# Starting the work area of SBUF 32 bytes later

## The reference

```python
for t in range(S):
    state = gamma * state + einsum('bhd,bhe->bhde', k[:, :, t], v[:, :, t])
    y[:, :, t] = scale * einsum('bhd,bhde->bhe', q[:, :, t], state)
x = y.transpose(0, 2, 1, 3).reshape(3072, 512)
h = x @ w_in                                  # 512 -> 2048
x = where(h > 0, h, exp(minimum(h, 0)) - 1) @ w_out
h = x @ w_in2                                 # 512 -> 1024
e = exp(h - max(h)); solu = h * e / (sum(e) + 1e-9)
out = (layer_norm(solu) * g_ln) @ w_out2      # 1024 -> 512
```

## Time and profile before

| | |
|---|---|
| time, median of 3 runs (lowest to highest) | 944.09 us (943.19 to 945.95) |
| span of the profiled execution | 942.4 us |
| TensorE busy | 925.3 us, 98% |
| VectorE, ScalarE, GpSimd busy | 44%, 37%, 12% |
| attention stage, up to the first L430 | about 115 us |
| first network | about 543 us |
| second network | about 285 us |

### The profile page before, as it was taken

One profiled execution on the slowest core, in us unless ns is written; L12 is line 12 of the kernel. 1 busy time (PEld: TensorE's weight loads), 2 busy tenths in 40 slices (PEclk: granted clock), 3 DMA queues, 4 the chain that ended last, 5 costly groups with the idle time before them and its releaser, 6 DMA issues.

```text
span 942.4 us, 13461 instructions
## 1 busy us (share of the span) xinstructions
PE 925.3 (98%) x4910; PEld 749.0 (79%) x4910; DVE 418.5 (44%) x826; ACT 346.4 (37%) x625; POOL 112.5 (12%) x147
## 2 busy tenths in 40 slices
PE   8898999999999999999999999999999999999998
PEld 5677788888888888888888888888888888888887
DVE  3555754432223222422332232246765666666663
ACT  2343565443334333433443334335322222222222
POOL 4455400000000000000000000014111111111110
PEclk9999999999999999999999999999999999999999
DMA  8777950000000000000000000210000000000000
GB/s 242 230 242 244 322 187 1 1 1 0 1 1 0 0 0 0 0 0 0 0 0 0 0 1 0 95 63 23 11 23 22 22 22 22 22 22 22 22 22 34
DMA packets 17818, 45.26 MB, mean 48 GB/s; under 512 B 2304, under 2 KB 2432, under 8 KB 17792
## 3 DMA queue, kind: packets, MB, share of 16 engines
q1 hardware_dynamic: 17072, 44.12, 13.9%
q10 hardware_dynamic: 720, 0.79, 0.3%
HBM read 38.61 MB, written 6.29 MB: 48 GB/s over the span
## 4 chain that ended last, share of the span: by engine, by line
PE 91%; DMA 6%; issue 1%; DVE 1%; POOL 0%; ACT 0%; SPq 0%; DVEq 0%; POOLq 0%; ACTq 0%
PE ps L430 10%; PE ps L451 10%; PE ps L450 10%; PE ps L454 10%; PE ps L436 10%; PE ps L431 9%; DMA tiles<-units_dram 5%; PE ps L509 4%; PE ps L511 4%; PE ps L510 4%; PE ps L480 4%; PE ps L481 4%; PE ps L482 4%; PE ps L496 2%; PE ps L365 2%; PE ps L389 2%
## 5 line engine op out<-in xcount | busy, mean ns | idle before, releaser
L633 DVE SCALAR_TENSOR_TENSOR e<-e,ps 128x512 f32<-128x512 f32 x96 | 65.8, 686 | 215.6 <-ACT e L809 215.6
L430 PE MATMUL ps<-x_hi,w_hi 128*128 128x512 f32 x384 | 152.4, 397 | 0.0
L450 PE MATMUL ps<-g_hi,w_hi 128*128 128x512 f32 x384 | 151.7, 395 | 0.0
L454 PE MATMUL ps<-g_lo,w_hi 128*128 128x512 f32 x384 | 151.7, 395 | 0.0
L451 PE MATMUL ps<-g_hi,w_lo 128*128 128x512 f32 x384 | 151.7, 395 | 0.0
L431 PE MATMUL ps<-x_hi,w_lo 128*128 128x512 f32 x384 | 151.1, 394 | 0.0
L638 DVE TENSOR_TENSOR g_lo<-e,g_hi 128x512 fp32r<-128x512 f32 x96 | 70.1, 730 | 128.8 <-ACT g_hi L815 128.6
L807 ACT ACTIVATE e<-ps 128x512 f32<-128x512 f32 x96 | 57.5, 599 | 164.8 <-PE ps L436 164.7
L815 ACT ACTIVATE g_hi<-e 128x512 fp32r<-128x512 f32 x96 | 60.8, 633 | 135.7 <-PE ps L454 126.2
L436 PE MATMUL ps<-x_lo,w_hi 128*128 128x512 f32 x384 | 105.0, 395 | 0.0
L430 PEld LDWEIGHTS ps<-x_hi,w_hi 128*128 128x128 f32 x384 | 72.0, 188 | 18.1 <-issue 0.2
(11 more groups left out here) (73 smaller groups left out, 1121.3 us busy)
## 6 DMA issues: line engine op xcount, KB each, us to landing
tiles<-units_dram SPq DMA_DIRECT2D x47, 512.0 KB, 4.3
w_raw<-w_dram SPq DMA_DIRECT2D x32, 256.0 KB, 6.6
out_dram<-y_sb SPq DMA_DIRECT2D x24, 256.0 KB, 2.0
w_raw<-w_in_dram SPq DMA_DIRECT2D x4, 512.0 KB, 4.6
w_raw<-w_out_dram SPq DMA_DIRECT2D x4, 512.0 KB, 3.3
mask_and_q_decay<-tables_dram ACTq DMA_DIRECT2D x3, 256.0 KB, 4.8
tiles<-units_dram SPq DMA_DIRECT2D x2, 256.0 KB, 3.3
ident<-tables_dram SPq DMA_DIRECT2D x1, 64.0 KB, 4.6
```

The source lines that it names most:

```text
L430: nc.tensor.matmul(bank, hi, x_hi[:, k, :], start=(k == 0), stop=False)
L450: nc.tensor.matmul(ps[:, 4 + m, :], hi, g_hi[:, f % 2, :], start=(f == 0), stop=False)
L454: last = nc.tensor.matmul(ps[:, 4 + m, :], hi, g_lo[:, f % 2, :], start=False, stop=(f == NF1 - 1))
```

## The change

One line is added in the layout, before the work area is placed. It rounds the next free address up to a multiple of 64 bytes. `WORK_AT` was 197536 and becomes 197568. No instruction, semaphore, size or order of work changes; every operand that lies in the work area has an address 32 bytes higher.

```diff
         WLO_AT = region(NW1 * 512 * 4)
         CONST_AT = region(800)
+        top[0] += -top[0] % 64
         WORK_AT = region(0)
```

## The result

The changed kernel takes 936.03 us (median of 4 runs, 933.08 to 936.75), the kernel before 945.02 us beside it. The ratio is 0.9905, with a 95% interval from 0.9882 to 0.9928: about 9 us less, where 19.6 were forecast. The time lies outside the stated range of 919 to 931.

A forecast was written before the change was run, and what follows sets the result against it. TensorE, busy for 98% of the span, was taken to bound the kernel through the distance between matmul starts. Gains of 15.3 + 2.7 + 0.6 + 1.0 = 19.6 us gave 944.1 - 19.6 = 924.5 us, range 919 to 931.

The forecast's parts named there:

- What bounds the kernel: Whole kernel: for some 825 of 942 us the time is the number of matmuls times the distance between starts.
- what would be late next: In the tiles and the first network, the faster matmuls were expected to uncover no wait for other engines.
- The mechanism: TensorE matmuls: an operand starting amid a 64-byte stretch needs one more stretch read, 6.6 ns per matmul.
- First network: All 2304 matmuls of the first network gain 6.6 ns each, 15.3 us, all on the path.
- `solu_up`: Second network, 23 tiles: 24 - 6 matmuls per tile gain 6.6 ns each, 2.7 us; tile 0 gains nothing.
- Transposes: 192 transposes whose stationary operand lies in the work area: between 0 and 1.3 us gained, 0.6 us taken.
- The six slow matmuls per tile: Six matmuls after each group of transposes keep 231.7 ns, so the second network gains 2.7 us, not 3.6.
- Attention: Attention stage, 1248 short matmuls with both operands in the work area: 0 to about 4.1 us gained, 1.0 taken.
- The region: Rival: position in SBUF or something else shared matters, not address; time stays 944.1 us; no change had 0.10 in all.
- The stretch of 128 bytes: Rival: any start off a multiple of 128 costs 6.6 ns, so time stays 944.1 us; no change had 0.10 in all.
- Only the moving operand gains: Rival: the first network's 15.3 us plus part of the attention gain remain, 928.3 us; chance 0.04.
- The rule of 16-byte lines: SBUF reads: both work area addresses are multiples of 16, so no extra crossing and 944.1 us; no change had 0.10.

The follow-up runs named there:

- work_at_128: Against the kernel before, the work area begins 32 bytes earlier, at 197504, with `mv` moved behind `bn`; 925.05 us, ratio 0.9803.
- weights_32_later: Against the kernel before, work area kept at 197536 while xT, both weight regions and constants move 32 bytes up; 926.63 us, ratio 0.9823.
- distance_192: Work area at 197568 as in the changed kernel, weights moved to 66304; 942.34 us, ratio 0.9984 to the kernel before.
- offsets: Separate small kernel without the computation: 49 groups of 48 matmuls, each with its own operand start addresses; 226.7 ns per matmul at 0, 233.3 at 32.

## Why the prediction was wrong

**What bounds the kernel: right.** TensorE is busy without a gap in the first network, and the gain arose there alone, as a shorter distance between starts. No new wait took anything back. In work_at_128, where starts are closest, the span is 18.5 us shorter, so what would be late next, judged from the earlier trace rows, was judged rightly.

**The mechanism: wrong, and this is the step that failed.** The prediction read 6.6 ns as the price of one more stretch of 64 bytes, paid by any operand off a multiple of 64. The sign and the place came out of it, and the paces of before fit it: 233.3 ns with the moving operand 32 bytes off, the same with the stationary one off, 226.5 with neither. By it `WORK_AT` on a multiple of 64 had to give 226.7 ns; it gave 229.0 in the first network and 233.8 in `solu_up`. What sets the pace is the distance between the two operands modulo 256: 0 gives 226.7 with nothing aligned to 64 (weights_32_later), and 192 gives 233.4 with the work area aligned (distance_192). In the trace of before all fast rows had both operands at the same phase modulo 256, and all slow ones had +32 or -32 between them. Alignment and distance never varied apart in that trace. The agreement with 16 columns was a coincidence of numbers that I took for evidence.

With the measured table the result can be worked out. The change moves the distance from 32 to 64 in the first network: 233.3 becomes 229.0. In `solu_up`, where the work area is the stationary side, it moves from -32 to -64, that is from 224 to 192 modulo 256: 233.1 and 233.1 in offsets.

**The terms.** First network: 15.3 us forecast, 10.0 measured, 2304 x 4.4 ns = 10.1. `solu_up`: 2.7 forecast, 0 measured. Both sizes would have been right for a distance of 0: work_at_128 gave 15.1 and 2.8. Transposes: 0.6 forecast, 0 measured, 0.79 us for eight before and after. The six slow matmuls per tile, kept in the forecast for `solu_up` on the strength of tile 0 and of a `solu_down` after transposes, came out in size; but those of tile 0 stand behind no transposes, and vanish in work_at_128. Attention: 1.0 forecast; all its buffers move together, so no distance changes, and by what the runs show it should gain nothing. The 1.4 us of the profiled execution are within the 4.3 us by which that stage differs among executions.

**Off the path.** L815 was to fall from 633 to 618 ns. It is unchanged:

```profile
L816 ACT ACTIVATE g_hi<-e 128x512 fp32r<-128x512 f32 x96 | 60.7, 632 | 131.3 <-PE ps L455 121.8 <-DVE e L634 9.5
```

It is 632 ns in work_at_128 too. The 15 ns between L763 and L815 have another cause, not looked for.

**The rivals.** The region is refuted by offsets. The stretch of 128 bytes is too: both at 32 is fast, and 128 against 0 is slow. "Only the moving operand gains" described the outcome best, but for a reason that is wrong, and with a size that was too large. None of the rivals named the relation between the two operands, so no weight could be given to a partial gain, and the range ended at 931. A rival made by asking what else the fast rows had in common would have been: both operands at the same phase; its price for a distance of 64 was unknown, between 0 and 15.3 us, and it would have widened the range to 944.

**The rule of 16-byte lines.** The Trainium skill's page "SBUF — State Buffer", section "Specifications (TRN2)", gives lines of 16 bytes and a penalty for each crossing. By it the change should do nothing. The measurement decides otherwise: at unchanged 16-byte alignment the pace goes from 226.7 to 233.3 ns and back.

**What stays open.** Whether the reads of the two operands share a resource, and which, why the period is 256 bytes, why the excess over 213.3 ns remains at distance 0, and why the first few matmuls after transposes, or after matmuls at another distance, are slow. The runs show that the pace depends on both addresses, that neither of the two pairings explains it alone, that the price of 32 over 0 shrinks from 6.6 to 1.0 ns with a stationary operand of 64 or 32 columns, and that none is seen with bf16 at the three distances tried.

## What to carry to other kernels

Where a stream of fp32r matmuls bounds a kernel, measure the distance between starts for each pair of operands and look at the addresses of both, modulo 256. For 512 moving and 128 stationary columns, lay both out at the same phase: 226.7 against 233.3 ns, 2% of this whole kernel. When a price in a trace goes with one property of the fast cases, list everything else that they share before taking it as the cause, and measure the two apart with a small kernel.

## What the runs showed of the hardware that was not expected

The start of one operand matters only against that of the other. For 512 columns of fp32r the pace in ns at a distance (moving minus stationary, modulo 256) of 0, 32, 64, 96, 128, 160, 192, 224 is 226.7, 233.3, 229.2, 233.5, 233.3, 234.2, 233.1, 233.1. At distances that are not a multiple of 8 bytes it can reach 240.0, at multiples of 8 up to 237.1 (at 168). The difference between 0 and 32 is 6.6 ns with 128 stationary columns, 2.7 with 96, and 1.0 with 64 and with 32. With 448 columns 64 is the best of the distances tried (200.0 against 202.5 at 0); with 384 columns 0, 32 and 64 do not differ; with bf16 the pace is 216.0 ns at 0 and 215.8 at 32. When the distance changes, up to eight or so starts pass before the new pace is reached.
